# First expert layer: turned rows and logit parts from one fp32 product per block

## The chip, the cores and the metric

The kernel runs on one core of one Trainium2 chip. The metric is the device time of one execution in microseconds (us); the median of three runs counts. All inputs and the output are fp32 in HBM.

## The reference

Gated linear attention, then two layers of experts with one expert per row.

```python
# attention, per batch b and head h (B=4, H=8, S=768, D=48), f = sigmoid(f_logit)
state = f[:, :, t, :, None] * state + np.einsum('bhd,bhe->bhde', k[:, :, t], v[:, :, t])
y[:, :, t] = np.einsum('bhd,bhde->bhe', q[:, :, t], state)
# rows of all heads side by side: x is 3072 x 384
# first layer (8 experts, F = 1024): expert by cosine to expert_emb, gate = softmax at that expert
out[mask] = gate_w[mask, None] * (np.maximum(x[mask] @ w1[e], 0.0) @ w2[e])
# second layer, x = output of the first
do_compute = x @ w_skip > 0
logits = xc @ w_gate                  # xc = x[do_compute], w_gate is 384 x 8
e_idx = np.argmax(logits, axis=1)     # gate_w = softmax(logits) at e_idx
y[mask] = gate_w[mask, None] * (np.maximum(xc[mask] @ w1[e], 0.0) @ w2[e])
out[do_compute] = xc + y
```

The change is where the first layer's result becomes input of the second: its rows are turned, and the 9 products w_gate and w_skip (8 logits and the skip score) are taken of them.

## The kernel before, in words

**Stages.** Attention works on 16 pairs of heads; its rows go to a table in HBM that is sorted by expert (sorted_rows), by indirect DMAs of GpSimd. VectorE then makes a plan of units (make_plan). Each expert layer loops over the experts and their units (over_experts, L273); every engine runs the same loops and reads the same plan. On these inputs the first layer has eight units, one for each expert: five with 384 rows (SMALL) and three with 448 (LARGE, three blocks of 128 rows and one of 64). The blocks are called slots, 0 to 3. Behind the last unit follows a tail without loops, then the plan and the units of layer two.

**A unit of the first layer on TensorE** (unit_mixed, L984). Every weight and activation is split into a high and a low part (fp32r), and a product is three: hi by hi, hi by lo, lo by hi. The expand part (expand_mixed, L940, matmuls L947 to L949) makes h in 8 blocks kf of 128 features, each over 3 blocks kd of the input. Its PSUM banks rotate over three (ps_h), so block kf waits for h_lo of block kf-3 (L990). The contract part (contract_mixed, L952, matmuls L956 to L958) makes the result with features on the partitions, for kd 0, 1, 2 (ps_yt), and ScalarE copies each to y_t (copy_y, L1238, activation L1241). In kd 1, after kf 4, TensorE takes the next unit's rows by transposes (take_mixed, L931).

**Routing runs one unit behind.** y_t of a unit is turned and routed in the next one, or in the tail for the last:
- route_logits (L963, matmul L970): 4 slots x 3 kd products in full fp32, y_t as the weights and the 9 gate columns (gate_w_t) as the moving side; kd 0 and 1 in the middle of contract kd 2 (L1008), kd 2 behind expand block 0 (L991). All three add up in ps_logit_u, in bank_u.
- turn_rows (L975, transposes L981): 4 slots x 3 kd transposes of y_t behind expand block 1 (L993), into ps_row, four banks.
- rank (L858), behind block 4, from the one-hot of the choice.

**The other engines in a unit.** ScalarE: high parts of the unit's w2 (split_hi, L1102), h_hi per block (L1248), softmax after block 4, high parts of the next expert's w1, the copies of y_t, x_hi of the next rows. VectorE: low parts of w2 (L1367), h_lo per block (L1719), after block 1 pick_rows (L1626: logits times gate, maximum, one-hot), after blocks 3 and 4 rows_to_send (L1651: turned rows times gate into row_send), after block 6 place_rows (L1677: the slot index), low parts of w1, x_lo (L1706). pick_rows is a Chain: each step waits for the one before it by a semaphore. GpSimd sends the rows by index to layer two's table and to out (L648, L653). SyncE loads the next rows (L452 to L456), the pads (L439), and the weights: w1 of the next expert (load_w1, L391) waits for the count of g["logit"], that is for the kd 2 logits of the unit.

**The tail** (L1024 on, ScalarE L1261, VectorE L1740): the kd 2 logits, turn slots 0 and 1, rank, turn slots 2 and 3; pick_rows, place_rows and the plan of layer two on VectorE; row copies on ScalarE with the softmax behind the first; the sends on GpSimd from slot_idx (L1695) on.

## Time and profile before

| what | us |
|---|---|
| three runs | 699.60, 699.98, 700.12; median 699.98 |
| the profiled execution | 697.99 |
| its span, first to last instruction | 696.2 |
| TensorE busy in matmuls | 652.9 (94%) |
| VectorE busy | 433.6 (62%) |
| ScalarE busy | 306.0 (44%) |
| GpSimd busy | 169.4 (24%) |
| mean granted TensorE clock | 0.969 of full speed |

The profile is that of the one profiled execution. Its own time is 1.8 us above its span. A line such as L947 is that of the kernel above. PE is TensorE, PEld its weight loads, DVE VectorE, ACT ScalarE, POOL GpSimd, SP SyncE. A matmul's duration in a row is from its start to its modelled end; matmuls overlap, so the time that one costs is read from the distance between starts. A product in full fp32 stands in the trace as two records, a transpose or an fp32r product as one.

### The profile page before, as it was taken

How to read it: one execution, taken by the hardware profiler on the slowest of the kernel's cores; microseconds unless marked ns; L12 is line 12 of the kernel's file. 1: busy time of each engine (PE TensorE's matmuls, PEld its weight loads, DVE VectorE, ACT ScalarE, POOL GpSimd, SP SyncE). 2: the span in 40 equal slices, each digit the busy share in tenths (PEclk: the TensorE clock that was granted, in tenths of full speed). 3: DMA queues.
4: the chain of work that ended last, by engine and by line, in shares of the span. 5: the costliest groups of instructions: out<-in, count | busy, mean ns of one | idle time of the engine just before them, and what ended most of it. 6: DMA issues, size and time to landing. Idle time of an engine off the chain costs nothing.

```text
span 696.2 us, 15659 instructions
## 1 busy us (share of the span) xinstructions
PE 652.9 (94%) x5042; PEld 624.7 (90%) x5043; DVE 433.6 (62%) x931; ACT 306.0 (44%) x514; POOL 169.4 (24%) x195
## 2 busy tenths in 40 slices
PE   5999999999839999999999999998499999999997
PEld 4989999999829999999899999997499999999997
DVE  5788888979444565738273838373276546557652
ACT  2665656656303433434243534332066436336640
POOL 5321244262430004040505042222401110110111
PEclk9999999999658999999999999999899999999999
DMA  9376876672133443617071717240376473464610
GB/s 186 71 150 137 195 184 149 125 173 52 58 119 118 167 160 124 227 61 255 33 249 35 249 36 266 66 184 19 92 279 211 144 256 125 155 226 147 237 41 23
DMA packets 144217, 100.68 MB, mean 145 GB/s; under 512 B 106319, under 2 KB 135098, under 8 KB 144176
## 3 DMA queue, kind: packets, MB, share of 16 engines
q1 hardware_dynamic: 137008, 87.42, 43.1%
q0 software_dynamic: 7168, 12.73, 5.1%
q8 instruction: 24, 0.39, 0.2%
q14 instruction: 17, 0.14, 0.1%
HBM read 79.46 MB, written 30.08 MB: 157 GB/s over the span
## 4 chain that ended last, share of the span: by engine, by line
PE 88%; issue 4%; DVE 3%; ACT 2%; DMA 1%; DVEq 1%; SPq 0%; POOL 0%; POOLq 0%
PE bank_a L947 7%; PE bank_a L949 7%; PE banks_y L819 7%; PE bank_a L948 7%; PE banks_s L798 4%; PE banks_y L956 4%; PE banks_y L958 3%; PE banks_y L957 3%; PE banks_y L970 3%; PE banks_y L811 3%; PE bank_b L947 2%; PE bank_b L948 2%; PE bank_b L949 2%; PE banks_y L749 2%; PE bank_b L956 2%
## 5 line engine op out<-in xcount | busy, mean ns | idle before, releaser
L1367 DVE TENSOR_TENSOR w_lo<-raw_w,w_hi 128x768 fp32r<-128x768 f32 x128 | 115.1, 952 | 45.6 <-ACT w_hi L1103 45.6
L1103 ACT ACTIVATE w_hi<-raw_w 128x768 fp32r<-128x768 f32 x128 | 99.2, 836 | 10.5 <-issue 10.5
L947 PE MATMUL bank_a<-x_hi,w_hi 128*128 128x384 f32 (+2 forms) x288 | 98.2, 341 | 3.6 <-issue 1.5
L949 PE MATMUL bank_a<-x_hi,w_lo 128*128 128x384 f32 (+2 forms) x288 | 95.4, 331 | 0.0
L948 PE MATMUL bank_a<-x_lo,w_hi 128*128 128x384 f32 (+2 forms) x288 | 95.4, 331 | 0.0
L648 POOL DMA_INDIRECT sorted_rows<-row_send,slot_idx x32 | 34.0, 1063 | 212.7 <-DVE slot_idx L1695 205.4
L658 POOL DMA_INDIRECT out<-row_send,out_idx x24 | 23.7, 987 | 173.6 <-DVE row_send L1762 157.7
L947 PEld LDWEIGHTS bank_a<-x_hi,w_hi 128*128 128x128 f32 x288 | 54.1, 188 | 8.8 <-issue 5.3
L949 PEld LDWEIGHTS bank_a<-x_hi,w_lo 128*128 128x128 f32 x288 | 54.1, 188 | 0.8
L948 PEld LDWEIGHTS bank_a<-x_lo,w_hi 128*128 128x128 f32 x288 | 54.2, 188 | 0.7
L1290 ACT ACTIVATE h_hi<-bank_a 128x384 fp32r<-128x384 f32 (+1 forms) x48 | 21.6, 450 | 73.9 <-PE bank_a L949 73.9
L819 PE MATMUL banks_y<-raw_v,scores 128*128 128x48 f32 x384 | 50.0, 282 | 0.0
L819 PEld LDWEIGHTS banks_y<-raw_v,scores 128*128 128x128 f32 x384 | 47.7, 200 | 1.2
L604 POOL TENSOR_SCALAR_AFFINE_SELECT scores<-scores 128x768 f32<-128x768 f32 x32 | 30.3, 947 | 75.1 <-ACT scores L1139 75.1
L1706 DVE TENSOR_TENSOR x_lo<-bank_a,x_hi 128x448 fp32r<-128x448 f32 x18 | 10.4, 620 | 60.1 <-issue 43.4
L956 PE MATMUL banks_y<-h_hi,w_hi 128*128 128x384 f32 (+1 forms) x128 | 45.3, 354 | 0.0
L958 PE MATMUL banks_y<-h_hi,w_lo 128*128 128x384 f32 (+1 forms) x128 | 44.5, 347 | 0.0
L957 PE MATMUL banks_y<-h_lo,w_hi 128*128 128x384 f32 (+1 forms) x128 | 44.4, 347 | 0.0
L1777 DVE SCALAR_TENSOR_TENSOR h_lo<-bank_a,h_hi 128x384 fp32r<-128x384 f32 (+1 forms) x48 | 24.3, 505 | 31.1 <-ACT h_hi L1290 29.1
L1139 ACT ACTIVATE scores<-banks_s 128x768 f32<-128x768 f32 x32 | 25.8, 806 | 33.5 <-PE banks_s L798 33.4
L1248 ACT ACTIVATE h_hi<-bank_a 128x384 fp32r<-128x384 f32 (+1 forms) x48 | 23.6, 506 | 37.9 <-PE bank_a L949 37.9
L653 POOL DMA_INDIRECT out<-row_send,out_idx x32 | 34.5, 1079 | 9.8 <-issue 9.1
(269 smaller groups left out, 1564.1 us busy)
## 6 DMA issues: line engine op xcount, KB each, us to landing
raw_w<-in_moe_w SPq DMA_DIRECT2D x30, 1536.0 KB
sorted_rows<-pad_row SPq DMA_DIRECT2D x8, 582.0 KB
raw_f<-in_f_logit SPq DMA_DIRECT2D x32, 144.0 KB, 3.2
raw_k<-in_k SPq DMA_DIRECT2D x32, 144.0 KB, 3.0
raw_q<-in_q SPq DMA_DIRECT2D x32, 144.0 KB, 3.6
raw_v<-in_v SPq DMA_DIRECT2D x32, 144.0 KB, 2.8
xs<-sorted_rows SPq DMA_DIRECT2D x11, 388.0 KB, 3.3
xs<-sorted_rows SPq DMA_DIRECT2D x19, 194.0 KB, 3.0
```

Of the source, the lines that this page charges most:

```text
L604: pool.affine_select(out=scores[:, half, :, :], in_=scores[:, half, :, :], compare_op=ALU.is_ge, fill=0.0, base=0, pattern=[[0, C], [1, P] ...
L648: pool.indirect_dma_start(sorted_rows[1], bass.IndirectOffsetOnAxis(ap=slot_idx[:, k:k + 1], axis=0), row_send[:, k, :], None, bounds_chec ...
L653: pool.indirect_dma_start(out, bass.IndirectOffsetOnAxis(ap=out_idx[:, k:k + 1], axis=0), row_send[:, k, 0:DM], None, bounds_check=N - 1, ...
L819: ins = pe.matmul(ps_y[h][:, c, :], scores[:, half, h * (C // 2) + c3, :], raw_v[par][:, c, h, :], start=False, stop=True, skip_group_chec ...
L947: pe.matmul(bank, hi, x_hi[:, kd, 0:size], start=(kd == 0), stop=False)
L948: pe.matmul(bank, hi, x_lo[:, kd, 0:size], start=False, stop=False)
L949: ins = pe.matmul(bank, lo, x_hi[:, kd, 0:size], start=False, stop=(kd == KD - 1))
L956: pe.matmul(bank, hi, h_hi[:, kf, 0:size], start=(kf == 0), stop=False)
L957: pe.matmul(bank, hi, h_lo[:, kf, 0:size], start=False, stop=False)
L958: return pe.matmul(bank, lo, h_hi[:, kf, 0:size], start=False, stop=(kf == KF - 1))
L1103: act.activation(w_hi[:, sl, :], raw_w[:, sl, :], ACT.Copy).then_inc(w_split_hi, 1)
L1367: dve.tensor_tensor(w_lo[:, sl, :], raw_w[:, sl, :], w_hi[:, sl, :].bitcast(F32), ALU.subtract).then_inc(w_split_lo, 1)
```

## The change

One tile turn_t (128 x 3 x 137) holds for each kd the 9 gate columns and behind them a 128 x 128 identity. One fp32 product per slot and kd, y_t as weights and turn_t[:, kd] as the moving side, gives 9 columns of partial logits and 128 of turned rows. Each kd writes columns of its own (start and stop at every product), three times 137 in one bank per slot (ps_turn). So the sum over kd is no longer made in PSUM: VectorE adds the three parts with three tensor_reduce (slots 0 and 1 together, 2, 3) into partial, and the scores are taken from there. The products that added up logits (route_logits) and the transposes (turn_rows as it was) go, and with them the zero matmul that opened the bank.

All 12 products stand behind expand block 0. Each slot's last product counts up f["turned"]; what waited for g["logit"] now waits for that count of all four slots, SyncE's loads too. In the tail six of them (kd 0 and 1 of slots 0, 1 and 3, EARLY_PARTS) stand ahead of the wait for the last copy of y_t, the other six behind it; rank follows, and ScalarE runs the softmax ahead of the four row copies. GpSimd fills the identities once at the start, before its memset of row_send; VectorE clears partial once. UNIT_STEPS goes from 19 to 22 for the three links more.

```diff
@@ -103,7 +103,9 @@
...
         emb_t = sb("emb_t", [P, KD, E])
-        gate_w_t = sb("gate_w_t", [P, KD, E + 1])
+        TURN = E + 1 + P
+        turn_t = sb("turn_t", [P, KD, TURN])
+        partial = sb("partial", [P, MIXED_SLOTS, E + 1])
         tau_col = sb("tau_col", [P, 1])
@@ -197,8 +199,9 @@
...
         ps_yt = [bank_y[:, 0:LARGE], bank_b[:, 512:512 + LARGE], bank_y[:, 0:LARGE]]
-        ps_row = [bank[:, 0:DM] for bank in (bank_s[0], bank_s[1], bank_y, bank_b[:, 512:1024])]
-        ps_logit_u = bank_u[:, 0:MIXED_SLOTS * 16].rearrange("p (c x) -> p c x", c=MIXED_SLOTS)
+        ps_turn = [bank[:, 0:KD * TURN].rearrange("p (k x) -> p k x", k=KD)
+                   for bank in (bank_s[0], bank_s[1], bank_y, bank_b[:, 512:1024])]
+        ps_turn_pair = banks_s[:].rearrange("p (c y) -> p c y", c=2)[:, :, 0:KD * TURN].rearrange("p c (k x) -> p c x k", k=KD)
         ps_rank_u = bank_u[:, 128:128 + MIXED_SLOTS * E].rearrange("p (c x) -> p c x", c=MIXED_SLOTS)
@@ -249,7 +252,7 @@
...
 
-        from_one_pe = [gs[1]["logit"]]
+        turned_at_start = MIXED_SLOTS
         from_one_act = [y_copied, exact_copied]
@@ -384,8 +387,8 @@
...
                 for kd in range(KD):
-                    sp.dma_start(gate_w_t[:, kd, 0:E], w_gate[kd * P:(kd + 1) * P, :]).then_inc(gate_in, 16)
-                    sp.dma_start(gate_w_t[:, kd, E:E + 1], w_skip[kd * P:(kd + 1) * P, :]).then_inc(gate_in, 16)
+                    sp.dma_start(turn_t[:, kd, 0:E], w_gate[kd * P:(kd + 1) * P, :]).then_inc(gate_in, 16)
+                    sp.dma_start(turn_t[:, kd, E:E + 1], w_skip[kd * P:(kd + 1) * P, :]).then_inc(gate_in, 16)
 
@@ -463,7 +466,7 @@
...
                                 settle(sp)
-                        sp.wait_ge(gs[1]["logit"], u + 1)
+                        sp.wait_ge(f["turned"], MIXED_SLOTS * u + turned_at_start)
                         settle(sp)
@@ -478,7 +481,7 @@
...
                                 second_weights()
-                            sp.wait_ge(gs[1]["logit"], u + 2)
+                            sp.wait_ge(f["turned"], MIXED_SLOTS * u + MIXED_SLOTS + turned_at_start)
                             settle(sp)
@@ -494,7 +497,7 @@
...
                     last = total_units(sp, 0)
-                    sp.wait_ge(gs[1]["logit"], last + 1)
+                    sp.wait_ge(f["turned"], MIXED_SLOTS * last + turned_at_start)
                     settle(sp)
@@ -588,6 +591,8 @@
...
 
+            pool.wait_ge(const_ready, 2)
+            ch.link(pool.tensor_copy(turn_t[:, :, E + 1:TURN], ident[:].rearrange("p (o x) -> p o x", o=1).to_broadcast((P, KD, P))))
             ch.link(pool.memset(row_send[:], 0.0))
@@ -711,8 +716,7 @@
...
         def _(pe):
-            for count in from_one_pe:
-                pe.sem_inc(count, 1)
+            pe.sem_inc(fs[0]["turned"], turned_at_start)
             pe.wait_ge(const_ready, 2)
@@ -960,26 +964,20 @@
...
 
-                def route_logits(u, kds, s=s):
-
-                    pe.wait_ge(s["y_copied"], KD * u + kds[-1] + 1)
-                    pe.wait_ge(g["slot"], u + 1)
-                    for kd in kds:
-                        for slot in range(MIXED_SLOTS):
-                            n = slot_rows(slot)
-                            ins = pe.matmul(ps_logit_u[0:n, slot, 0:E + 1], y_t[:, kd, slot * P:slot * P + n], gate_w_t[:, kd, :],
-                                            start=(kd == 0 and slot == 0), stop=(kd == KD - 1), skip_group_check=True)
-                    if kds[-1] == KD - 1:
-                        ins.then_inc(g["logit"], 1)
-
-                def turn_rows(u, slots, s=s):
+                def turn_rows(u, parts, copied, s=s):
 
                     pe.wait_ge(s["row"], MIXED_SLOTS * u + 3)
-                    for slot in slots:
+                    pe.wait_ge(s["y_copied"], KD * u + copied)
+                    for kd, slot in parts:
                         n = slot_rows(slot)
-                        for kd in range(KD):
-                            ins = pe.transpose(ps_row[slot][0:n, kd * P:(kd + 1) * P], y_t[:, kd, slot * P:slot * P + n], ident[:])
-                        ins.then_inc(s["turned"], 1)
+                        ins = pe.matmul(ps_turn[slot][0:n, kd, :], y_t[:, kd, slot * P:slot * P + n], turn_t[:, kd, :],
+                                        start=True, stop=True)
+                        if kd == KD - 1:
+                            ins.then_inc(s["turned"], 1)
+
+                ALL_PARTS = [(kd, slot) for slot in range(MIXED_SLOTS) for kd in range(KD)]
+                EARLY_PARTS = [(kd, slot) for slot in (0, 1, 3) for kd in range(2)]
+                LATE_PARTS = [part for part in ALL_PARTS if part not in EARLY_PARTS]
 
@@ -989,9 +987,7 @@
...
                         if kf == 0:
-                            route_logits(u, (2,))
-                        if kf == 1:
-                            turn_rows(u, range(MIXED_SLOTS))
+                            turn_rows(u, ALL_PARTS, KD)
                         if kf == 4:
@@ -1005,14 +1001,9 @@
...
                                 take_mixed(u + 1)
-                            if kd == 2 and kf == 4:
-                                route_logits(u + 1, (0, 1))
                         ins.then_inc(s["y"], 1)
...
                 if m == 0:
-                    pe.matmul(ps_logit_u, zeros[:], zeros[:, 0:MIXED_SLOTS * 16].rearrange("p (c x) -> p c x", c=MIXED_SLOTS),
-                              start=True, stop=True)
-
                     def first_rows():
@@ -1023,10 +1014,9 @@
...
                     last = total_units(pe, 0)
-                    route_logits(last, (2,))
-                    turn_rows(last, (0, 1))
+                    turn_rows(last, EARLY_PARTS, 2)
+                    turn_rows(last, LATE_PARTS, KD)
                     rank(g, last + 1, MIXED_SLOTS, ps_rank_u, ps_count_u)
-                    turn_rows(last, (2, 3))
                     pe.wait_ge(s["x_lo"], KD * last + KD)
@@ -1259,14 +1249,13 @@
...
                     last = total_units(act, 0)
+                    softmax(g, last, MIXED_SLOTS)
                     for slot in range(MIXED_SLOTS):
...
                         act.wait_ge(rows_sent, last + 1)
-                        act.wait_ge(s["turned"], MIXED_SLOTS * last + slot + 1)
-                        act.activation(row_send[0:n, slot, 0:DM], ps_row[slot][0:n, :], ACT.Copy,
+                        act.wait_ge(s["turned"], MIXED_SLOTS * last + slot + 1 + turned_at_start)
+                        act.activation(row_send[0:n, slot, 0:DM].rearrange("p (k x) -> p k x", k=KD), ps_turn[slot][0:n, :, E + 1:TURN], ACT.Copy,
                                        scale=kept[0:n, slot, 0:1]).then_inc(s["row"], 1)
-                        if slot == 0:
-                            softmax(g, last, MIXED_SLOTS)
                     continue
@@ -1320,6 +1309,7 @@
...
             ch.link(dve.memset(worst[:], 1.0))
+            ch.link(dve.memset(partial[:], 0.0))
             for m in range(2):
@@ -1327,7 +1317,7 @@
...
             ROUTE_A = 19
-            UNIT_STEPS = (19, 3)
+            UNIT_STEPS = (22, 3)
 
@@ -1631,8 +1621,13 @@
...
                 ch.link(dve.tensor_scalar(real, tokens, float(N), None, ALU.is_lt))
-                dve.wait_ge(g["logit"], u + 2)
-                ch.link(dve.tensor_tensor(scored[:], ps_logit_u[:, :, 0:E + 1],
+                dve.wait_ge(fs[0]["turned"], MIXED_SLOTS * u + MIXED_SLOTS + turned_at_start)
+                ch.link(dve.tensor_reduce(partial[:, 0:2, :], ps_turn_pair[:, :, 0:E + 1, :], AX.X, ALU.add))
+                for slot in range(2, MIXED_SLOTS):
+                    n = P if slot < SLOTS else HB
+                    ch.link(dve.tensor_reduce(partial[0:n, slot, :], ps_turn[slot][0:n].rearrange("p k x -> p x k")[:, 0:E + 1, :],
+                                              AX.X, ALU.add))
+                ch.link(dve.tensor_tensor(scored[:], partial[:],
                                           gates.rearrange("p (c o) -> p c o", o=1).to_broadcast((P, nt, E + 1)), ALU.mult))
@@ -1654,8 +1649,8 @@
...
                     n = P if slot < SLOTS else HB
-                    dve.wait_ge(s["turned"], MIXED_SLOTS * u + slot + 1)
-                    dve.tensor_scalar(row_send[0:n, slot, 0:DM], ps_row[slot][0:n, :], kept[0:n, slot, 0:1], None,
+                    dve.wait_ge(s["turned"], MIXED_SLOTS * u + slot + 1 + turned_at_start)
+                    dve.tensor_scalar(row_send[0:n, slot, 0:DM].rearrange("p (k x) -> p k x", k=KD), ps_turn[slot][0:n, :, E + 1:TURN], kept[0:n, slot, 0:1], None,
                                       ALU.mult).then_inc(s["row"], 1)
...
             def keep_fresh(ch, next_u):
```

On TensorE, around expand blocks 0 and 1 of a unit with 384 rows, before (L970: logit products, L981: transposes; expand matmuls shortened to one triple of three):

```order
L949 MATMUL bank_a<-x_hi,w_lo 128x384
L966 REGISTER_ALU
L970 MATMUL banks_y<-gate_w_t,y_t 128x9 x3
L970 MATMUL banks_y<-gate_w_t,y_t 64x9
L947 MATMUL bank_a<-x_hi,w_hi 128x384
L948 MATMUL bank_a<-x_lo,w_hi 128x384
L949 MATMUL bank_a<-x_hi,w_lo 128x384
...
L977 ISA
L981 MATMUL banks_s<-ident,y_t 128x128 x6
L981 MATMUL banks_y<-ident,y_t 128x128 x3
L981 MATMUL bank_b<-ident,y_t 64x128 x3
```

and of the change (expand is L951 to L953 there):

```order
L953 MATMUL bank_a<-x_hi,w_lo 128x384
L969 ISA
L973 MATMUL banks_s<-turn_t,y_t 128x137 x6
L973 MATMUL banks_y<-turn_t,y_t 128x137 x3
L973 MATMUL bank_b<-turn_t,y_t 64x137 x3
L951 MATMUL bank_a<-x_hi,w_hi 128x384
L952 MATMUL bank_a<-x_lo,w_hi 128x384
L953 MATMUL bank_a<-x_hi,w_lo 128x384
```

Both groups have become one, all of it ahead of block 1. In the contraction of kd 2 stood before (and stands no more; the contract matmuls now follow each other there):

```order
L958 MATMUL banks_y<-h_hi,w_lo 128x384
L965 ISA
L970 MATMUL banks_y<-gate_w_t,y_t 128x9 x3
L970 MATMUL banks_y<-gate_w_t,y_t 64x9
L970 MATMUL banks_y<-gate_w_t,y_t 128x9 x3
L970 MATMUL banks_y<-gate_w_t,y_t 64x9
L956 MATMUL banks_y<-h_hi,w_hi 128x384
```

On VectorE, the head of pick_rows of the change, behind h_lo of block 1 (the rows ISA and REGISTER_ALU are waits):

```order
L1714 SCALAR_TENSOR_TENSOR h_lo<-bank_a,h_hi 128x384
L1623 TENSOR_SCALAR cols<-kept 128x4
L49 ISA
L1624 ISA
L1625 TENSOR_REDUCE partial<-banks_s 128x18
L49 REGISTER_ALU
L1628 TENSOR_REDUCE partial<-banks_y 128x9
L49 REGISTER_ALU
L1628 TENSOR_REDUCE partial<-bank_b 64x9
L49 REGISTER_ALU
L1630 TENSOR_TENSOR scored<-partial,kept 128x36
```

Before, scored followed the first row directly, from banks_y (L1635); the three reductions are new.

## Rows read from the trace of the kernel before

**Rows 1.** Page, chain of work that ended last, by engine

```profile
PE 88%; issue 4%; DVE 3%; ACT 2%; DMA 1%; DVEq 1%; SPq 0%; POOL 0%; POOLq 0%
```

**Rows 2.** Waits of PE, 210 to 495 us: waiter, releaser, total, times, longest

```profile
PE bank_a L947 <- issue: 1.5, 3, 0.7
```

**Rows 3.** Timeline of PE in contract kd 2: start us, us, engine, line, operation

```profile
275.87 1.92 PE L970 MATMUL banks_y<-gate_w_t,y_t 128*128 128x9 f32 x16
...
278.00 0.34 PE L957 MATMUL banks_y<-h_lo,w_hi 128*128 128x384 f32 x1
```

**Rows 4.** Timeline of PE behind expand block 0

```profile
250.10 0.94 PE L970 MATMUL banks_y<-gate_w_t,y_t 128*128 128x9 f32 x8
...
251.26 0.34 PE L948 MATMUL bank_a<-x_lo,w_hi 128*128 128x384 f32 x1
```

**Rows 5.** Timeline of PE behind expand block 1

```profile
252.65 0.82 PE L981 MATMUL banks_s<-ident,y_t 128*128 128x128 f32 x6
...
254.13 0.34 PE L948 MATMUL bank_b<-x_lo,w_hi 128*128 128x384 f32 x1
```

**Rows 6.** Timeline of PE in attention, fp32 products with 128 and 48 columns

```profile
123.52 0.94 PE L798 MATMUL banks_s<-q_down,k_up 64*128 64x128 f32 x12
124.35 1.34 PE L811 MATMUL banks_y<-state,q_down 64*128 64x48 f32 x20
125.62 1.54 PE L819 MATMUL banks_y<-raw_v,scores 128*128 128x48 f32 x12
127.00 0.40 PE L719 MATMUL banks_s<-ident,raw_f 128*128 128x128 f32 x2
```

**Rows 7.** Timeline of DVE in the same unit, pick_rows and the h_lo behind it

```profile
255.91 0.20 DVE L1635 TENSOR_TENSOR scored<-banks_y,kept 128x36 f32<-128x36 f32 x1
256.14 0.19 DVE L1637 TENSOR_REDUCE cols<-scored 128x4 f32<-128x32 f32 x1
...
257.99 0.56 DVE L1719 SCALAR_TENSOR_TENSOR h_lo<-bank_b,h_hi 128x384 fp32r<-128x384 f32 x1
```

**Rows 8.** Timeline of PE, first matmul of expand block 5

```profile
258.87 0.42 PE L947 MATMUL bank_b<-x_hi,w_hi 128*128 128x384 f32 x1
```

**Rows 9.** Timelines of SP's queue and of ACT: w1 issued, and its split begun

```profile
252.95 0.38 SPq L391 DMA_DIRECT2D raw_w<-in_moe_w  x1
...
264.22 0.84 ACT L1103 ACTIVATE w_hi<-raw_w 128x768 fp32r<-128x768 f32 x1
```

**Rows 10.** Window: length, busy PE PEld DVE ACT POOL, PEclk, DMA share, GB/s

```profile
252.95:258.25 5.30, 5.30 (x36) 5.30 (x35) 4.72 (x17) 2.17 (x5) 0.00 (x0) 1.00 0.98 310
```

**Rows 11.** Timelines of DVE and PE: last x_lo, first matmul of the next unit

```profile
275.50 0.61 DVE L1706 TENSOR_TENSOR x_lo<-bank_b,x_hi 128x448 fp32r<-128x448 f32 x1
...
279.61 0.43 PE L947 MATMUL bank_a<-x_hi,w_hi 128*128 128x384 f32 x1
```

**Rows 12.** Chain that ended last, behind the last unit: start us, us, what

```profile
480.63 0.55 ACT y_t L1241
481.31 1.06 PE banks_y L970 x8
482.39 0.21 DVE scored L1635
```

**Rows 13.** Timeline there, the slot index and the first send

```profile
485.89 0.17 DVE L1695 TENSOR_SCALAR slot_idx<-cols 128x4 uint32<-128x4 f32 x1
...
486.95 0.98 POOL L648 DMA_INDIRECT sorted_rows<-row_send,slot_idx  x1 [11.59 <-DVE slot_idx L1695]
```

**Rows 14.** Timeline at the start of the program, DVE and POOL

```profile
7.40 1.48 DVE L1340 COPY start_inv<-inv_f 128x6 f32<-128x6 f32 x1
7.46 1.39 POOL L591 MEMSET row_send<- 128x1552 f32 x1
```

**Rows 15.** Windows behind the first layer, columns as in rows 10

```profile
486.00:494.00 8.00, 0.45 (x8) 0.30 (x6) 4.26 (x28) 0.00 (x0) 5.53 (x6) 0.73 0.40 134
...
498.00:504.00 6.00, 3.58 (x40) 3.16 (x41) 1.49 (x3) 1.26 (x3) 0.00 (x0) 1.00 0.27 71
```

## The prediction, made before the changed kernel was timed

> **What bounds the kernel now.** I read the page first, then the waits of the stretch that the change touches, then TensorE's timeline around the changed products, then the other engines at the same places. TensorE holds 88% of the chain that ended last [rows 1]. From 210 to 495 us, which is the whole first expert layer, it stood idle in front of a matmul of an expert block three times, 1.5 us in all [rows 2]. So inside the eight units of this layer a microsecond of TensorE work taken out is a microsecond won, until some other engine's result comes too late. Behind the last unit it is different: there the chain leaves TensorE for VectorE [rows 12].
>
> **What the parts cost on TensorE today.** I take the time that a group takes out of the stream: from its first record to the second matmul behind it, less the 0.17 us of one ordinary step. That matters because the first ordinary matmul behind short ones waits longer for its weights.
> - Logit products of kd 0 and 1, in the middle of the last contraction: 16 records, 275.87 to 278.00, so 2.13 - 0.17 = 1.96 us [rows 3].
> - Logit products of kd 2, behind the first expand block: 8 records, 250.10 to 251.26, so 0.99 us [rows 4]. One product in full fp32 is two records here, about 0.122 us each.
> - The turning, behind the second block: 12 transposes of one record each, 252.65 to 254.13, so 1.31 us, 0.109 us each at 128 columns [rows 5].
> Together 4.26 us in each unit.
>
> **What takes their place.** Twelve fp32 products, so 24 records, of 137 columns. No such record is in the trace, so I bound it. From below: no record of a full 128 x 128 weight block comes faster than the transposes' 0.109 us, and 24 of them are 2.62 us. From above: load and stream one after the other, 0.122 (the 9-column record, nearly all load) + 0.117 = 0.239 us, 5.74 us in all. Two rows say that it lies low. The records with 48 columns take (127.00 - 125.62) / 12 = 0.115 us, no longer than those with 9, so streaming lies beside loading [rows 6]. And the 64-row products with 128 columns need 0.84 us for 12 records in six pairs on separate halves of the array, at most 0.14 us per record even if both of a pair run fully beside each other [rows 6]. I take the transposes' 0.109 us grown with the columns: 0.109 x 137/128 = 0.117 us, 24 x 0.117 = 2.81 us. A unit then wins 4.26 - 2.81 = 1.45 us, eight units **11.6 us**. The one zero matmul that goes lies in a wait: nothing.
>
> **VectorE.** Before the scores three reductions are added (54 and twice 27 elements in). Neighbours in the same linked chain follow each other by 0.22 to 0.24 us [rows 7], so +0.68 us; all of it delays the third h_lo, which TensorE needs for the sixth expand block. Before, that h_lo ended at 257.99 + 0.56 = 258.55 and the block began at 258.87: 0.32 us spare [rows 7, 8]. Now the block comes 2.81 - 0.99 - 1.31 = 0.51 us later in its unit, the h_lo 0.68 us later, and some 0.1 us more because the second expand block now ends 1.82 us later and its h_hi reaches VectorE just behind the weight splits. What is spare is 0.32 + 0.51 - 0.78 = 0.05 us. I book 0.1 us of waiting in each of the five units with 384 columns, **-0.5 us**; those with 448 have longer blocks and more to spare. The row scaling reads the same 384 elements, in three pieces: nothing.
>
> **SyncE.** The load of the next expert's w1 waited for the kd 2 logits and now waits for all turned slots: 2.81 - 0.99 = 1.82 us later. It was issued at 252.95, and ScalarE split it from 264.22 on with no idle time [rows 9]. From the issue to 258.25 the queues moved 310 GB/s x 5.3 us = 1.64 MB [rows 10]; w1 has 1.57 MB and shares the stretch with the pads, so at that rate both (2.2 MB) are there after 7 us, at 260, some 4 us early. 1.82 us later is covered; with the cover gone each unit would lose what is over. The row load and w2 behind it on the queue move by as much; the rows are not needed before the middle of the next-to-last contraction, w2 not before the next unit.
>
> **The next unit's start.** TensorE reaches it 1.96 us earlier after the take. x_lo is ready at 276.11 (L1706: 275.50 + 0.61), the block began at 279.61, now at 277.65: still 1.5 us to spare [rows 3, 11].
>
> **The end of the layer.** Here the saving turns round. Before, the last 8 records began at 481.31, when ScalarE had copied y_t, and the scores at 482.39 [rows 12]. Now all 24 records stand there, 12 of them before that copy. They can begin at some 480.8 (the copy of y_t begins at 480.63, at the end of the last contraction [rows 12]), so they end near 483.6; with 0.68 us of reductions the scores begin near 484.4 to 484.8, +2.0 to +2.4 us. Everything behind is a chain from the scores over slot_idx (485.89) to the first send (486.95) [rows 13], so it moves as one: **-2.2 us**. ScalarE's row copies now stand behind the softmax, but the first row needs only that and one copy, and slot_idx comes 3.5 us after the scores.
>
> **The start.** GpSimd gets a copy of 384 elements before its long memsets; its chain ends under a microsecond later, before anyone needs it. But VectorE's copy of six columns took 1.48 us, from 7.40 to the end of the row_send memset at 8.85 [rows 14]. With the turn_t copy in that memset's place it may be let through earlier or later: between 0.6 us won and 0.9 us lost. I book nothing. The Trainium skill (SBUF — State Buffer, "SBUF: two separate sides") says that VectorE and GpSimd share a port pair that one of them holds for a whole instruction; the 1.48 us agree, and by that rule the shorter copy in front would win the 0.6.
>
> **Sum.** 11.6 - 0.5 - 2.2 = 8.9 us. The profiled execution took 697.99 us, 2.0 under the median of the three runs, and would take 689.1; on the median of 699.98 that is **691.1 us**. The measurement can tell about 0.2%, 1.4 us, from no change.
>
> **Rivals.**
> 1. *VectorE's chain becomes the bound in every unit* (0.12). If each reduction costs twice my price, because it gathers across three pieces of two banks, 0.05 us spare become 0.6 us of waiting in five units, and the end loses 0.7 us more: 8.9 - 2.7 - 0.7 = 5.5 us won, 694.5. For it: no row reads PSUM so scattered. Against: the 36 scores come from PSUM in a 16-column stride at 0.20 us [rows 7].
> 2. *The fp32 record costs load plus stream* (0.06). At 0.239 us a unit loses 5.74 - 4.26 = 1.48 us, eight lose 11.8, the end 2.2 + 24 x 0.122 = 5.1: 717 us, slower. It decides from about 0.160 us per record: there the units win 8 x (4.26 - 3.84) = 3.4 us and the end loses 3.2. Against it both of [rows 6]. The Trainium skill ("TensorE: Matmul & The Clock Gate", Terms, the xbus row) calls transpose mode four times faster for FP32, and "FP8 and Floating Point Precision", TensorE Precision Notes, says that true FP32 takes four passes; a product would be four transposes. As rows: 4 x 0.117 x 12 = 5.6 us, nearly the same case. The pairs of 128-column records speak against it, since two records of such a product take 0.28 us and not 0.44.
> 3. *The freed time is not on the path* (0.08): a late w1, or the splits, hold the next unit, and the saving shrinks to the end's loss. Then 8.9 falls to between -2.2 and +2, about 700 us. Against: no such wait is in [rows 2], and I find 1.5 us and more spare at each.
> 4. *The clock* (0.04). It is at the lower of its two levels (1.2 GHz) while TensorE idles behind the layer, 0.73 on average from 486 to 494 us, and back at full speed from 498 on [rows 15], before layer two's first block. A longer idle time before the scores could carry that into layer two; 10 us at half speed cost 5 us: 696.
>
> **How the numbers follow.** The forecast has 0.70. Its own spread: records at 0.109 us give 1.5 us more, the start 0.6; records at 0.125 us and a later end take 2 us. The low end, 688.5, is the lower bound of the record; the high end, 696.5, takes in rivals 1 and 4. Left out are rivals 2 and 3, 0.14. Faster by over 0.2%: 0.70 + 0.12 + 0.04 + a fourth of rival 3 = 0.88. Within: 0.04. Slower: 0.08, rival 2 and the rest of rival 3.
>
> **What would show it.** A turn group of 24 records in about 2.8 us behind the first block, no records in the third contraction, units shorter by 1.4 us; TensorE not waiting for h_lo before the sixth block; w1 split without idle; scores beginning about 4 us behind the end of the last contraction instead of 1.8. A group of over 3.8 us, or a wait for h_lo over 0.5 us, would prove me wrong.

## The result, and the profile after

| | before | changed |
|---|---|---|
| median, same chip, 16 runs each | 703.27 us | 696.05 us |
| ratio, 95% interval | | 0.9913 [0.9894, 0.9933] |
| profiled execution (its span) | 697.99 (696.2) | 698.73 (697.0) |
| first unit of layer one starts at | 217.21 | 224.52 |
| first unit to the last contraction matmul (8 units) | 263.03 | 252.19 |
| from there to layer two's first expand matmul | 23.08 | 26.86 |
| layer two to the end of the span | 192.88 | 193.43 |

The changed kernel is faster by 0.9% (6.1 us at this interval's middle, on 700; the two medians alone would give 0.9897). Forecast were 691.1 on 699.98, a ratio of 0.9873; 0.9913 lies 0.4% above it. The two profiles hide even that, since their executions differ before layer one by more than the change gains. So I read stage by stage. The units won what was forecast (-10.84 us, booked -11.1). The time is lost at the two ends: 3.8 us behind the last unit, where 2.2 were booked, and in this pair of profiles 7.3 us ahead of the first, where nothing was booked. That last number is not a price: the experiments show how far single profiles vary there.

TensorE's timeline of the changed kernel, the second unit of layer one, around the new group (start us, us, engine, line, operation):

```profile
255.96 1.57 PE L973 MATMUL banks_s<-turn_t,y_t 128*128 128x137 f32 x12
257.37 0.86 PE L973 MATMUL banks_y<-turn_t,y_t 128*128 128x137 f32 x6
258.16 0.92 PE L973 MATMUL bank_b<-turn_t,y_t 128*64 128x137 f32 x6
259.01 0.44 PE L951 MATMUL bank_a<-x_hi,w_hi 128*128 128x384 f32 x1
259.29 0.34 PE L952 MATMUL bank_a<-x_lo,w_hi 128*128 128x384 f32 x1
...
265.58 0.42 PE L951 MATMUL bank_b<-x_hi,w_hi 128*128 128x384 f32 x1
```

This one group stands for [rows 3 to 5]. By the same rule as there it takes 259.29 - 255.96 - 0.17 = 3.16 us: not the 2.81 booked, but 1.10 us less than the 4.26 of before. The lines show where the 0.35 sits. The first 12 records, 255.96 to 257.37, are 0.1175 us each, the price booked. The 6 ahead of the fourth slot, to 258.16, are 0.132 each. The fourth slot's 6, with 64 weight columns (128\*64), to 259.01, are 0.142 each. The step out of the group is 0.28 us instead of 0.17. Before, the turning had three such records too, and they cost 0.24 us together, no more than the others:

```profile
253.63 0.49 PE L981 MATMUL bank_b<-ident,y_t 128*64 128x128 f32 x3
253.87 0.42 PE L947 MATMUL bank_b<-x_hi,w_hi 128*128 128x384 f32 x1
```

The start of a unit, on the same timeline as in [rows 11], holds a second gain that I had not seen. Before, the next unit's first matmul began 0.39 us behind the last of the contraction, at 279.61:

```profile
279.22 0.34 PE L958 MATMUL banks_y<-h_hi,w_lo 128*128 128x384 f32 x1
```

Now:

```profile
283.96 0.34 PE L962 MATMUL banks_y<-h_hi,w_lo 128*128 128x384 f32 x1
284.14 0.34 PE L951 MATMUL bank_a<-x_hi,w_hi 128*128 128x384 f32 x1
```

It is 0.18 us instead of 0.39 here, and 0.48 to 0.52 instead of 0.98 to 1.0 at two others. Over the seven boundaries that gives 2.0 us, and with 8 x 1.10 the 10.8 of the table. A unit of 384 columns goes from 31.21 to 29.85 us.

VectorE in the same unit, as in [rows 7]:

```profile
262.17 0.21 DVE L1625 TENSOR_REDUCE partial<-banks_s 128x18 f32<-128x54 f32 x1
262.42 0.19 DVE L1628 TENSOR_REDUCE partial<-banks_y 128x9 f32<-128x27 f32 x1
262.64 0.18 DVE L1628 TENSOR_REDUCE partial<-bank_b 64x9 f32<-64x27 f32 x1
262.85 0.20 DVE L1630 TENSOR_TENSOR scored<-partial,kept 128x36 f32<-128x36 f32 x1
...
264.93 0.56 DVE L1714 SCALAR_TENSOR_TENSOR h_lo<-bank_b,h_hi 128x384 fp32r<-128x384 f32 x1
```

The three reductions cost 262.85 - 262.17 = 0.68 us, exactly as booked. The third h_lo ends at 265.49 and its block begins at 265.58: 0.09 us spare where I had 0.05. TensorE's waits from 218 to 480 us hold no h_lo:

```profile
PE bank_a L951 <- DVE x_lo L1701: 0.7, 1, 0.7
PE bank_a L951 <- issue: 0.2, 1, 0.2
```

Behind the last unit, against [rows 12, 13], first the last contraction matmul of the kernel before:

```profile
480.24 0.36 PE L958 MATMUL banks_y<-h_hi,w_lo 128*128 128x448 f32 x1
```

and from the timelines of the changed kernel (TensorE, VectorE, GpSimd):

```profile
476.71 0.36 PE L962 MATMUL banks_y<-h_hi,w_lo 128*128 128x448 f32 x1
...
481.09 0.20 DVE L1630 TENSOR_TENSOR scored<-partial,kept 128x36 f32<-128x36 f32 x1
...
484.59 0.17 DVE L1690 TENSOR_SCALAR slot_idx<-cols 128x4 uint32<-128x4 f32 x1
...
485.64 0.98 POOL L653 DMA_INDIRECT sorted_rows<-row_send,slot_idx  x1 [11.80 <-DVE slot_idx L1690]
...
500.59 1.51 PE L1033 MATMUL bank_a<-ident,xs 128*128 128x128 f32 x6 [1.73 <-DMA xs<-sorted_rows]
501.90 0.85 PE L1033 MATMUL bank_b<-ident,xs 128*128 128x128 f32 x3
...
503.57 0.56 PE L951 MATMUL bank_a<-x_hi,w_hi 128*128 128x256 f32 x1
```

The scores begin 4.38 us behind the last contraction matmul; before it was 482.39 - 480.24 = 2.15. That is +2.23, the booked 2.2. From the scores to slot_idx it is 3.50 us as before, and to the send 4.55. But layer two begins 22.48 us behind the scores, and 20.93 before.

Ahead of layer one the profile's page itself tells, in the last column of its DMA part (median us from the issue of a transfer to its landing). The kernel before:

```profile
raw_f<-in_f_logit SPq DMA_DIRECT2D x32, 144.0 KB, 3.2
raw_k<-in_k SPq DMA_DIRECT2D x32, 144.0 KB, 3.0
raw_q<-in_q SPq DMA_DIRECT2D x32, 144.0 KB, 3.6
raw_v<-in_v SPq DMA_DIRECT2D x32, 144.0 KB, 2.8
```

and the changed kernel:

```profile
raw_f<-in_f_logit SPq DMA_DIRECT2D x32, 144.0 KB, 4.2
raw_k<-in_k SPq DMA_DIRECT2D x32, 144.0 KB, 4.4
raw_q<-in_q SPq DMA_DIRECT2D x32, 144.0 KB, 4.8
raw_v<-in_v SPq DMA_DIRECT2D x32, 144.0 KB, 2.9
```

No line of the diff touches these transfers, and their bytes are the same. Two windows of the attention stage (columns as in [rows 10]) say it again, first before, then changed: the DMA engines' busy share rises from 0.83 to 1.29 and from 0.56 to 0.76, while the bytes moved change by 5 to 7%.

```profile
0.00:20.00 20.00, 12.46 (x84) 10.68 (x87) 12.14 (x19) 7.37 (x10) 10.82 (x37) 1.00 0.83 163
100.00:180.00 80.00, 78.59 (x955) 74.10 (x957) 67.91 (x130) 48.74 (x72) 32.43 (x34) 0.99 0.56 123
```

```profile
0.00:20.00 20.00, 11.62 (x70) 9.68 (x72) 11.12 (x19) 6.81 (x9) 10.89 (x38) 1.00 1.29 155
100.00:180.00 80.00, 78.83 (x934) 74.13 (x934) 69.42 (x121) 50.02 (x74) 33.23 (x35) 1.00 0.76 131
```

### The profile page after: what moved, and what is told of

Its sections match the earlier page's. It is cut to its first block, busy times and chain, and to the rows that moved or that the text cites. A ratio compares the mean times of both kernels' runs of the same rounds, so it can differ in the third digit from the quotient of the medians.

```text
span 697.0 us, 15516 instructions
## 1 busy us (share of the span) xinstructions
PE 652.4 (94%) x4949; PEld 622.7 (89%) x4950; DVE 436.8 (63%) x959; ACT 306.7 (44%) x514; POOL 169.2 (24%) x196
## 4 chain that ended last, share of the span: by engine, by line
PE 85%; SPq 4%; issue 4%; DMA 3%; DVE 2%; ACT 1%; DVEq 0%; POOL 0%; POOLq 0%; ACTq 0%
PE bank_a L951 7%; PE bank_a L952 7%; PE bank_a L953 7%; PE banks_y L823 6%; PE banks_s L802 3%; PE banks_y L962 3%; PE banks_y L960 3%; PE banks_y L961 3%; PE bank_b L951 2%; PE bank_b L952 2%; PE bank_b L953 2%; PE banks_y L815 2%; PE banks_s L973 2%; PE banks_y L753 2%; PE bank_b L961 2%
## 5 line engine op out<-in xcount | busy, mean ns | idle before, releaser
L951 PE MATMUL bank_a<-x_hi,w_hi 128*128 128x384 f32 (+2 forms) x288 | 98.1, 340 | 1.5 <-DVE x_lo L1701 0.7
L953 PE MATMUL bank_a<-x_hi,w_lo 128*128 128x384 f32 (+2 forms) x288 | 95.5, 332 | 0.0
L653 POOL DMA_INDIRECT sorted_rows<-row_send,slot_idx x32 | 34.0, 1062 | 203.9 <-DVE slot_idx L1690 196.5
L951 PEld LDWEIGHTS bank_a<-x_hi,w_hi 128*128 128x128 f32 x288 | 54.4, 189 | 6.7 <-issue 4.2
L953 PEld LDWEIGHTS bank_a<-x_hi,w_lo 128*128 128x128 f32 x288 | 54.3, 189 | 0.9
L1279 ACT ACTIVATE h_hi<-bank_a 128x384 fp32r<-128x384 f32 (+1 forms) x48 | 21.6, 450 | 73.8 <-PE bank_a L953 73.8
```

Source lines behind the costliest of these rows:

```text
L653: pool.indirect_dma_start(sorted_rows[1], bass.IndirectOffsetOnAxis(ap=slot_idx[:, k:k + 1], axis=0), row_send[:, k, :], None, bounds_chec ...
L951: pe.matmul(bank, hi, x_hi[:, kd, 0:size], start=(kd == 0), stop=False)
L953: ins = pe.matmul(bank, lo, x_hi[:, kd, 0:size], start=False, stop=(kd == KD - 1))
```

## The experiments

**before_again, after_again**: both kernels once more, unedited, for the spread of the stages.

> The kernel before, once more, to see how far two executions of one kernel lie apart and where. Theory A (the 7 us by which the changed kernel's profile reached the expert layer later are not the change's, but waits for transfers in attention that come and go): another profile of this kernel can reach the first unit anywhere between 217 and 225 us, with units of 31.2 us each and again about 22.7 us from the last contraction to layer two. Rival (it is the change): every profile of this kernel reaches it near 217 us.

> The changed kernel once more, on the same chip. Theory A: units of 29.8 us at 384 rows again, the first unit anywhere from 217 to 225 us; from the end of the last contraction to layer two 26 us if the loss there is fixed (scores 4.0 us behind the contraction), or nearer 25 us if the 1.5 us behind the scores were chance. Time 6 to 9 us under the kernel before. Rival (the change slows attention): first unit again near 224 us.

Measured: ratios 0.9993 [0.9975, 1.0011] and 0.9916 [0.9893, 0.994]. Each unit came out within 0.05 us of its first profile (31.19 and 29.84 for the first). The stages around them did not: the first unit began at 220.8 in both. Single profiles can't price the start; the landings can, 3.1 us for raw_f before and 4.1 now, again.

**kd_inner**: the group's order turned, so that the weight width changes three times there and back, not once.

```
-                ALL_PARTS = [(kd, slot) for slot in range(MIXED_SLOTS) for kd in range(KD)]
+                ALL_PARTS = [(kd, slot) for kd in range(KD) for slot in range(MIXED_SLOTS)]
```

> The 12 products of a unit in the order kd outside, slot inside, so that TensorE goes to the 64-column weights of slot 3 three times and back three times instead of once. Theory B (the group costs 3.16 us and not 2.81 because each change between 128 and 64 columns of weights costs some 0.1 us): about 3.6 us for the group, units longer by 0.4 us, the whole 3 to 4 us slower than the changed kernel. Rival (the 0.35 us lie at the group's ends only): group unchanged at 3.2 us, time the same.

Measured: 0.9983 [0.9965, 1.0001]; the group takes 3.83 us, and six of the eight units are 0.65 to 0.68 us longer (the first 30.50). That is 0.33 us for each of the two added ways from 128 weight columns to 64 and back, where the theory had 0.2. Its group, on TensorE's timeline:

```profile
225.38 0.40 PE L973 MATMUL banks_y<-turn_t,y_t 128*128 128x137 f32 x2
225.71 0.45 PE L973 MATMUL bank_b<-turn_t,y_t 128*64 128x137 f32 x2
226.08 0.73 PE L973 MATMUL banks_s<-turn_t,y_t 128*128 128x137 f32 x4
```

Two records from 225.71 to 226.08 take 0.37 us where two at 0.117 would take 0.23. A change of order with no instruction more or less ate most of the gain.

**early_in_units**: six of the products moved back into the contraction before, the other six left behind the first expand block.

```
+                            if kd == 2 and kf == 4:
+                                turn_rows(u + 1, EARLY_PARTS, 2)
...
-                            turn_rows(u, ALL_PARTS, KD)
+                            turn_rows(u, LATE_PARTS, KD)
...
```

> Six of a unit's 12 products (kd 0 and 1 of slots 0, 1, 3) are moved back into the contraction of kd 2, behind kf 4, where the logit products stood in the kernel before; so the tail has only the other six. Theory C (the 0.26 us of idle time at each unit's start in the kernel before came from the short products shortly ahead of the unit's loop branch, and went with them): the gap of 0.2 us and more returns at the units' starts, and with a second pair of group ends units are 0.4 to 0.6 us longer, 3 to 5 us in eight units; the scores after the last contraction begin 1.2 us earlier than in the changed kernel; in all 2 to 4 us slower. Rival (the gap has to do with the number of records, or with waits): no gap, units as long as in the changed kernel, and the time 1 us better.

Measured: 1.0016 [0.9996, 1.0036]. Its two groups take 1.74 + 1.75 = 3.49 us instead of 3.16, and now the PE waits for VectorE:

```profile
PE bank_b L951 <- DVE h_lo L1716: 1.5, 4, 0.4
PE bank_a L951 <- DVE h_lo L1716: 1.0, 3, 0.5
```

The whole group behind the first block is what gives VectorE time for the splits and the choice. Three of the unit boundaries stayed at 0.17 to 0.18 us although short products stand in the last contraction again (the two longest went from 0.5 to 0.65), so these are not what made them 0.39 to 1.0 before; that reason of mine fell.

**aligned**: one unused tile. turn_t and partial together moved every tile allocated behind them, the attention's inputs among them. raw_f0 stood at byte 116032 of a partition, 64 behind a multiple of 256, and now at 117728, 224 behind one. Its rows are 192 bytes every 256, those of two heads in turn, so that the transfer of one head writes a row every 512.

```
+        pad_to_line = sb("pad_to_line", [P, 24])
         tau_col = sb("tau_col", [P, 1])
```

> The changed kernel with one unused tile of 96 bytes per partition ahead of tau_col, which moves every tile behind it. In the kernel before, raw_f0 begins at byte 116032 of a partition (64 behind a multiple of 256), so each row of 48 fp32 numbers (192 bytes) that an attention transfer writes ends exactly at the next multiple of 256. In the changed kernel turn_t and partial push it to 117728 (224 behind one), and every row crosses one; the pad puts it back to 64 behind. Theory A (the shifted addresses slow the attention's transfers, and that is the part of the loss that lies ahead of the first unit): raw_f, raw_k and raw_q land after 3.1, 3.0 and 3.7 us as in the kernel before, not after 4.2, 4.4 and 4.8; the first transposes begin 0.5 us earlier (4.3 us, not 4.84); the first unit of layer one starts 1 to 4 us earlier than the 222.8 us mean of the four profiles of changed kernels so far; units as after (29.85 and 34.1 us); median 1 to 3 us below the changed kernel's ratio of 0.992, so 0.988 to 0.990. Rival R (the transfers are slower for another reason of the new start, POOL's copy into turn_t or the loads of the gates in 9-number rows of a wider tile): landings stay at 4.2 to 4.8 us and the ratio at 0.992. Rival S (the landings return, but the attention stage hides them): landings 3.1 us, first transposes at 4.3 us, ratio still 0.992.

Measured: **0.9849 [0.9819, 0.9878]**, and the landings are back:

```profile
raw_f<-in_f_logit SPq DMA_DIRECT2D x32, 144.0 KB, 3.2
raw_k<-in_k SPq DMA_DIRECT2D x32, 144.0 KB, 3.2
raw_q<-in_q SPq DMA_DIRECT2D x32, 144.0 KB, 3.5
```

Units (29.84) and the end of the layer (26.64 us) are those of the changed kernel, and the DMA engines' share from 100 to 180 us is 0.56 again; rivals R and S fall. A second thing changed at the start. VectorE's copy, which took 1.48 us in the kernel before and 1.32 in the changed one, came ahead of GpSimd's copy here (7.39 us) and took 0.17, on VectorE's timeline:

```profile
7.32 0.17 DVE L1331 COPY start_inv<-inv_f 128x6 f32<-128x6 f32 x1
```

**before_shifted**: the kernel before with 160 unused bytes at the same place.

```
+        shift_by = sb("shift_by", [P, 40])
         tau_col = sb("tau_col", [P, 1])
```

> The kernel before with one unused tile of 160 bytes per partition, which puts raw_f0 at byte 116192, 224 behind a multiple of 256 as in the changed kernel; nothing else is changed. Theory A: raw_f, raw_k and raw_q land after 4.2 to 4.8 us instead of 3.0 to 3.7, the first unit starts 1 to 4 us later than 219 us, and the kernel is 1 to 3 us slower than the kernel before (ratio 1.002 to 1.004). Rival R (it is something else of the changed start): landings at 3.1 us, ratio 1.000. Rival S: landings at 4.2 to 4.8 us, ratio 1.000.

Measured: **1.0077 [1.0047, 1.0107]**, about 5 us lost by one declaration. Its page and TensorE's timeline:

```profile
raw_f<-in_f_logit SPq DMA_DIRECT2D x32, 144.0 KB, 4.2
raw_k<-in_k SPq DMA_DIRECT2D x32, 144.0 KB, 4.6
raw_q<-in_q SPq DMA_DIRECT2D x32, 144.0 KB, 5.0
```

```profile
4.65 1.51 PE L720 MATMUL banks_s<-ident,raw_f 128*128 128x128 f32 x6 [4.65 <-DMA raw_f<-in_f_logit]
8.20 1.54 PE L720 MATMUL bank_b<-ident,raw_k 128*128 128x128 f32 x6 [2.03 <-DMA raw_q<-in_q]
```

and the same two of the padded kernel:

```profile
4.17 1.52 PE L724 MATMUL banks_s<-ident,raw_f 128*128 128x128 f32 x6 [4.17 <-DMA raw_f<-in_f_logit]
6.91 1.54 PE L724 MATMUL bank_b<-ident,raw_k 128*128 128x128 f32 x6 [1.22 <-DMA raw_q<-in_q]
```

The theory had the direction right and the size too small in both. The cause is shown from both sides: the addresses alone make the kernel before slower and the changed one faster. Where the time goes in the stage is visible for its first 2 us: raw_k's transposes begin at 8.20 against 6.91, the second pair's first transpose at 11.58 against 9.67. In all seven profiles with raw_f0 at 224 it begins 6.9 us behind the first pair's, in all seven at 64 or 0 after 4.8 to 5.5. How the other 3 us are spread over the later pairs I can't tell from these profiles. Nor does an edit here move the attention's inputs alone, but pad_to_zero gives the other tiles behind them a third offset.

**pad_to_zero**: 32 bytes instead of 96, so raw_f0 on a multiple of 256.

```
+        pad_to_line = sb("pad_to_line", [P, 8])
```

> The changed kernel with a pad of 32 bytes instead of 96: raw_f0 at 117760, a multiple of 256 itself. Theory A1 (what counts is only that a 192-byte row doesn't cross a multiple of 256): landings of raw_f, raw_k and raw_q at 3.1 to 3.6 us and the ratio at 0.985 as with the pad of 96 bytes. Theory A2 (a row that begins on the multiple also saves the 64 bytes ahead of it): landings below 3.0 us, ratio below 0.985. Rival A3 (the gain of the 96-byte pad came from another tile behind it: the weights, the sent rows, the rows of the attention's output, which now stand elsewhere): landings at 3.1 to 3.6 us but the ratio at 0.99.

Measured: 0.9847 [0.9811, 0.9882], landings 3.3, 3.0 and 3.7 us. That is A1: what counts is that a row doesn't cross the multiple. A3 fell with the ratio. The Trainium skill (DMA: Bandwidth & Descriptors, "How a descriptor splits into AXI transactions") says that a transaction begins at a multiple of 256 bytes, and a row that begins elsewhere takes one from the multiple below it. It words this for reads, while the rows that moved here are written. By that rule, which makes this an estimate, a row at 224 takes two transactions and a row at 0 or 64 takes one, which fits the slower landings. By its beats a row at 0 should also be cheaper than one at 64 (6 against 8, an estimate too), and the runs don't show that.

**full_slot3**: the fourth slot's products also load 128 weight columns.

```
-        y_t = sb("y_t", [P, KD, LARGE])
+        y_t = sb("y_t", [P, KD, MIXED_SLOTS * P])
...
-                        n = slot_rows(slot)
+                        n = P
```

> The changed kernel with y_t 512 columns wide, so that the fourth slot's three products also load 128 weight columns (64 of them unused) and no product has another weight width than the one ahead of it. Theory B (the 0.35 us by which the new group exceeds 24 records of 0.117 us is paid at the change from 128 to 64 weight columns and back): the group takes 2.83 us instead of 3.16. The units of 448 rows become 0.3 us shorter (33.8 us). In the units of 384 rows the third h_lo was ready only 0.09 us before the PE wanted it, so they become 0.1 us shorter and the PE shows waits for h_lo of some 0.2 us. Rival: the 0.35 us belongs to the group's entry and exit, whatever the widths: the group stays at 3.1 to 3.2 us. The span falls by some 1.5 us by the theory and not by the rival. (y_t is 768 bytes longer, so the addresses behind it keep their place within 256 bytes.)

Measured in one execution, so without an interval: 691.49 us (span 689.7 against 692.0 and 697.0). TensorE's timeline:

```profile
221.45 1.57 PE L973 MATMUL banks_s<-turn_t,y_t 128*128 128x137 f32 x12
222.86 0.87 PE L973 MATMUL banks_y<-turn_t,y_t 128*128 128x137 f32 x6
223.57 0.86 PE L973 MATMUL bank_b<-turn_t,y_t 128*128 128x137 f32 x6
224.18 0.43 PE L951 MATMUL bank_a<-x_hi,w_hi 128*128 128x384 f32 x1
224.45 0.34 PE L952 MATMUL bank_a<-x_lo,w_hi 128*128 128x384 f32 x1
```

224.45 - 221.45 - 0.17 = 2.83 us, to the hundredth what the theory said: twice as many weight columns, and faster. The 448 units are 0.37 us shorter. In the 384 units h_lo came too late here and there (0.7 us in two waits), and they gained from nothing to 0.34 us. Eight units: 250.3 us. Behind the last unit the scores come 3.89 us behind the last contraction matmul instead of 4.38, a gain that I had not forecast.

**reduce_by_slot**: VectorE waits slot by slot.

```
-                dve.wait_ge(fs[0]["turned"], MIXED_SLOTS * u + MIXED_SLOTS + turned_at_start)
+                dve.wait_ge(fs[0]["turned"], MIXED_SLOTS * u + 2 + turned_at_start)
...
+                    dve.wait_ge(fs[0]["turned"], MIXED_SLOTS * u + slot + 1 + turned_at_start)
```

> The changed kernel, but the VectorE's three reductions each wait only for the slots that they read, not for all four. Theory (behind the last unit the scores are late by the whole group plus the reductions, so overlapping them gives time back): scores 0.4 to 0.5 us earlier behind the last contraction matmul (3.9 us instead of 4.38), layer two as much earlier; nothing changes in the units, where the group is over before VectorE comes to it. Rival (the rank matmuls or the row copies end last in the tail): scores earlier, layer two starts no earlier than 22.1 us behind the old place of the scores.

Measured in one execution: 693.35 us. The scores come 3.90 us behind the last contraction matmul (4.38 without), and layer two 26.23 us behind it instead of 26.5 to 26.9. That "nothing changes in the units" was wrong: from its first instruction to the scores the choice takes 1.16 us instead of 0.97, and 0.19 us is more than the 0.09 spare. TensorE waited once for h_lo (0.3 us), the first 384 unit went from 29.84 to 30.00, and all eight from 252.1 to 252.9.

**later_pick, combined, combined_warm**: the pad and the full width, with VectorE's choice one block later; then also slot by slot; then also keep-warm matmuls (short ones whose result nobody reads) ahead of the wait for the one-hot rows.

```
-                        if kf == 4:
+                        if kf == 5:
                             rank(g, u + 1, MIXED_SLOTS, ps_rank_u, ps_count_u)
...
-                        if kf == 1:
+                        if kf == 2:
                             pick_rows(ch, u)
```

> The changed kernel with three edits: the pad of 96 bytes (addresses as in the kernel before), the fourth slot's products with 128 weight columns, and VectorE's choice of rows behind the third h_lo instead of the second, with the rank products behind the sixth expand block instead of the fifth. Theory (in the 384 units the group's end no longer sets the pace alone; with the full width VectorE's third h_lo came 0.3 us too late, since it stood behind the 3.1 us of the choice): the PE shows no wait for h_lo in layer one, all 384 units become 0.33 us shorter than in the changed kernel (29.5 us from 29.84), the 448 units 0.37 (33.8); with the pad the ratio is 0.9849 minus 8 x 0.34 us, so 0.981, some 2.7 us below the padded kernel. Rival (the wait only moves to the fourth h_lo or to the rank products, which want the one-hot rows): waits for h_lo or onehot_b of 0.2 us or more in each 384 unit, ratio 0.984 as the padded kernel.

> The kernel with the pad, the full width and the later choice, and also VectorE's reductions waiting slot by slot. By itself that edit brought the scores 0.5 us earlier behind the last unit but made the 384 units 0.15 us longer, since VectorE's chain is 0.14 us longer there and the third h_lo stood behind it. Theory: with the choice moved behind the third h_lo that price is gone and the tail's 0.5 us stays: ratio 0.0007 below the kernel without it (too little for the interval; the profile is to show the tail at 25.7 to 26.2 us between the last contraction matmul and layer two, and the units as in the kernel without it). Rival: units 0.1 us longer again, no difference in sum.

> As the combined kernel, with 3 x the smallest block of keep-warm matmuls on the PE behind the last unit's group, while it waits 2.5 us for the one-hot rows. It tests whether the longer idle of the PE behind the scores (2.5 us against 1.0 in the kernel before) is what lets the clock fall from about 478 to 499 us, where the kernel before had it low for 7 to 10 us only. Theory W (it is that idle): the granted clock stays up until the plan of layer two, and the block between the rows' transposes and layer two's first product takes 2.64 us instead of 2.75 to 2.98: 0.1 to 0.5 us won. Rival (the clock falls in the later wait for the first rows of layer two): the same stretches of half clock, the same time, or up to 0.5 us lost where the keep-warm matmuls delay the rank products.

Measured: 0.9848 [0.9814, 0.9882], **0.9802 [0.9776, 0.9829]** and 0.9827 [0.9793, 0.9861]. In later_pick the wait for h_lo is gone, but not to the units' gain: they sum to 251.8 us, 1.4 more than with the full width alone, and the ratio is 0.985 and not the theory's 0.981. Two of them wait for the copy of y_t at the group, which ScalarE began late for a reason that its queue doesn't show:

```profile
PE banks_s L974 <- ACT y_t L1232: 1.3, 2, 0.7
```

The combined kernel is the fastest run here, about 14 us below the kernel before. Its interval just overlaps that of the padded kernel, and its units are not shorter (252.6 us), so its profile shows 1 us of advantage, at the end of the layer (25.57 us), and no more. Of the keep-warm matmuls the rival was right in the main: the idle time before the rank products shrank from 2.1 to 0.4 us, and the granted clock stayed up for 10.7 us behind the last contraction matmul instead of 7.1, but it still fell, and fell again in the wait for layer two's rows. Its first transposes for layer two (494.0 to 496.7 us) ran at 0.50, those of the combined kernel (491.7 to 493.5) at full speed.

## Why the prediction was right and wrong

**The step that failed is the start.** "I book nothing" weighed VectorE's copy alone, and in the changed kernel that came out at 1.32 us instead of 1.48: small, as said. What I did not ask is what else a new tile does. turn_t and partial moved everything allocated behind them by 1696 bytes, 224 instead of 64 behind a multiple of 256. That made 96 of the attention's transfers slower. I had the row (page, DMA part) and no reason to think that it would change. Its price: aligned against after_again is 0.0067 of 700, 4.7 us, give or take 2.7 (the two were measured on different chips, each against the kernel before), and before_shifted against before 5.4 us, [3.3, 7.5]. The bare profiles overlap: the first unit begins at 219.8 to 224.5 us in the seven with raw_f0 at 224, and at 212.5 to 220.8 in the seven at 64 or 0. They part once one interval is left out, picked after the fact because it varied most: from the seventh to the eighth run of the attention's score products (in the kernel before L798, and from 78.5 to 90.1 us), while the first expert's weights are loaded. It took 11.6 to 15.3 us, in both kernels. Without it the first unit begins at 207.1 to 209.9 us at 224, and at 200.8 to 206.9 at 64 or 0.

**Without the shift the total comes near the forecast, and that is in part luck**: 0.9873 forecast, 0.9849 [0.9819, 0.9878] measured with the pad. That is 10.6 us on 700, but the stages that the prediction priced account for less. With the pad the units take 251.9 us instead of 263.0, and from the last contraction matmul to layer two it is 26.6 to 26.9 instead of 22.7 to 23.8, so some 7.6 us in all. The other 3 us (the 10.6 are uncertain by 2.1 to either side) must lie for the most part ahead of the first unit. With the interval above left out it begins there at 203.9 us on average in the five padded profiles, against 205.7 and 206.9 in the two of the kernel before at the same place; at 224 at 208.4 on average in the six of the changed kernels, against 209.7 in before_shifted. So the new start seems to win 1 to 3 us besides what the shift costs. One part is that copy of VectorE's, for which I had weighed 0.6 us won: it took 0.17 to 0.36 us in all five padded profiles, and the first transposes of k_up began at 12.1 to 12.2 us instead of 13.2 to 13.3. With the shift it came later and took 1.32 again, so a part of the shift's 4.7 us goes this way. The rest stays open, and no run isolates either.

- *Units*: 11.6 - 0.5 = 11.1 us booked, 10.8 measured, but out of other parts. The record was right (0.117). The group was 0.35 us dearer, 2.8 in all, because I priced all 24 records alike, and the fourth slot's have another weight width; kd_inner and full_slot3 show it. The transposes that the price was taken from did not show it: their three narrow records cost 0.08 us each. The boundaries gave 2.0 back, unbooked; their cause stays open. The h_lo stall (0.5) did not come, by 0.09 us. [rows 2] leave out one wait, 0.7 us for x_lo at the first unit; it is the same before and after and changes no sum.
- *The end*: scores 2.23 us later, 2.2 booked. Behind them I took the chain to "move as one", and from the scores to layer two it took 22.1 to 22.5 us instead of 20.9, 21.6 and, in before_shifted, 20.6. From the first transpose to layer two's first block it is 2.74 to 2.98 us instead of 2.64 to 2.66, and 2.94 and more only where all the transposes ran at half the clock: six then take 500.59 to 501.90, 1.31 us, against 0.68 in the kernel before (500.68 to 501.36). That is rival 4's mechanism at less than a tenth of its size; layer two itself is as long as before, within the 1.4 us by which all profiles differ. The rest lies between the first send and the issue of layer two's rows: 11.7 to 11.8 us in all eleven profiles of changed kernels, and 10.6, 11.5 and 10.0 before. That stays open.
- *VectorE*: 0.68 us booked and measured; rival 1's price per reduction was wrong. Its mechanism is real, though: early_in_units, reduce_by_slot and full_slot3 each pushed VectorE over the edge and paid.
- *Rival 2*, four passes or load plus stream, fell: 0.117 us per record, two records per product, as [rows 6] said. *Rival 3* fell: w1's split (270.93) had no idle time that reached TensorE.

## What to carry to other kernels

A change that declares a tile also moves every tile behind it. Before pricing its instructions, compare the addresses of the transfers' targets against the multiples of 256 bytes, and afterwards look at the landing times of transfers that the diff does not touch. Price short products by the weight width as well as by their columns, and keep those of one width together. Where a kernel has 0.1 us to spare between two engines, every saving on one of them must be read at the other.

## What the hardware showed that I had not expected

- Rows of 192 bytes at a pitch of 256: 3.0 to 3.8 us to landing where they don't cross a multiple of 256 bytes, 4.1 to 5.0 where each does. raw_v, whose rows stand every 192 bytes, so that half of them cross before and three in four after, stayed at 2.7 to 3.0; why it is spared stays open.
- fp32 products of 137 columns: 0.117 us per record between equals; each way from 128 to 64 weight columns and back 0.33 us more, where three transposes of 64 weight columns cost nothing more. Loading 64 unused weight columns was cheaper than leaving them out.
- Half the clock doubled the time of six transposes (0.68 to 1.31 us), and 30 small matmuls behind the last group put its fall off (from 7.1 to 10.7 us behind the last contraction matmul) and did not hold it up through the wait for layer two's rows.
